# Attention beside an MLP: copies ahead of fades, the second fade of the quads two slots later, y of chunk 0 one slot later

## The reference

```python
# attention: B, H, S, D = 4, 8, 768, 48
f = 1.0 / (1.0 + np.exp(-f_logit))
for t in range(S):
    state = f[:, :, t, :, None] * state + np.einsum('bhd,bhe->bhde', k[:, :, t], v[:, :, t])
    y[:, :, t] = np.einsum('bhd,bhde->bhe', q[:, :, t], state)
# first MLP: x is y as 3072 tokens of 384, w_in 384 x 2048, w_out 2048 x 384
h = x @ w_in
x2 = (h * (1.0 / (1.0 + np.exp(-1.702 * h)))) @ w_out
# second MLP: E = 4 experts, w1 384 x 1024, w2 1024 x 384, p the shares of the experts
for e in range(E):
    out += p[:, e:e + 1] * (np.maximum(x2 @ w1[e], 0.0) @ w2[e])
```

## Time and profile before

| | us |
|---|---|
| median of 3 runs | 1386.29 |
| lowest, highest | 1384.8, 1388.15 |
| the profiled execution, its own time | 1386.22 |
| its span, first to last instruction | 1384.5 |
| TensorE busy, share | 1338.0, 97% |
| VectorE, ScalarE, GpSimd busy | 889.9, 570.7, 635.4 |

### The profile page before, as it was taken

The page is one execution under the profiler, slowest core; times in us unless marked ns, Lnnn a source line. Parts: engine busy times, 40 slices in busy tenths (PEclk is TensorE's granted clock), DMA queues, the critical chain, the costliest instruction groups (busy, mean ns, idle before and its releaser), DMA issues.

```text
span 1384.5 us, 26477 instructions
## 1 busy us (share of the span) xinstructions
PE 1338.0 (97%) x10837; PEld 1239.0 (89%) x10837; DVE 889.9 (64%) x1354; ACT 570.7 (41%) x975; POOL 635.4 (46%) x721
## 2 busy tenths in 40 slices
PE   6889999999999999999999999999999999999999
PEld 5789898989989898998999999999999999999998
DVE  8785848474757565456666666666666666666666
ACT  5564545454544444344333333333323434333331
POOL 8686666665656556466222122121211644444330
PEclk9999999999999999999999999999999999999999
DMA  9535252524343340122101010100101112222111
GB/s 158 120 80 91 69 73 70 71 72 61 82 50 93 41 103 4 63 69 63 35 23 35 13 35 12 35 23 24 35 13 58 46 47 69 70 69 69 57 47 46
DMA packets 240200, 79.34 MB, mean 57 GB/s; under 512 B 189136, under 2 KB 238544, under 8 KB 240080
## 3 DMA queue, kind: packets, MB, share of 16 engines
q1 hardware_dynamic: 201680, 74.11, 22.7%
q10 hardware_dynamic: 38400, 3.55, 2.1%
HBM read 67.83 MB, written 9.78 MB: 56 GB/s over the span
## 4 chain that ended last, share of the span: by engine, by line
PE 79%; DVE 9%; POOL 5%; issue 3%; ACT 2%; DMA 1%; SPq 0%; ACTq 0%; DVEq 0%; POOLq 0%
PE bank L1914 10%; PE bank L1912 10%; PE bank L1913 10%; PE bank L1848 9%; PE bank L1849 9%; PE bank L1847 9%; PE bank L1820 3%; PE bank L1821 3%; PE bank L1822 3%; PE bank L1632 3%; PE bank L1579 2%; PE bank L1577 2%; PE bank L1578 2%; PE bank L1588 2%; POOL g_l L832 2%
## 5 line engine op out<-in xcount | busy, mean ns | idle before, releaser
L1526 DVE SCALAR_TENSOR_TENSOR acc<-bank,p_n,acc 128x384 f32<-128x384 f32 x384 | 234.7, 611 | 68.1 <-PE bank L1914 63.0
L1914 PE MATMUL bank<-w_h,h_l 128*128 128x384 f32 x768 | 257.2, 335 | 0.0
L1912 PE MATMUL bank<-w_h,h_h 128*128 128x384 f32 x768 | 257.0, 335 | 0.0
L1913 PE MATMUL bank<-w_l,h_h 128*128 128x384 f32 x768 | 256.9, 334 | 0.0
L832 POOL TENSOR_TENSOR g_l<-sig,g_h 128x384 fp32r<-128x384 f32 x128 | 151.0, 1180 | 177.6 <-ACT g_h L1084 177.5
L1510 DVE TENSOR_TENSOR bank<-bank,x_copy 128x512 f32<-128x512 f32 x192 | 124.6, 694 | 166.0 <-ACT x_copy L1183 102.6
L1849 PE MATMUL bank<-xs,we_l 128*128 128x512 f32 x528 | 206.4, 391 | 0.0
L1848 PE MATMUL bank<-xs,we_h 128*128 128x512 f32 x528 | 206.2, 391 | 0.0
L1847 PE MATMUL bank<-xs,we_h 128*128 128x512 f32 x528 | 205.5, 389 | 0.6 <-issue 0.6
L882 POOL TENSOR_TENSOR we_l<-we_raw,we_h 128x384 fp32r<-128x384 f32 x96 | 97.1, 1038 | 214.9 <-ACT we_h L1151 214.9
L1183 ACT ACTIVATE x_copy<-bank 128x512 f32<-128x512 f32 x144 | 86.3, 599 | 221.8 <-PE bank L1849 221.5
(11 more groups left out here) (156 smaller groups left out, 2412.3 us busy)
## 6 DMA issues: line engine op xcount, KB each, us to landing
we_raw<-in_moe_w SPq DMA_DIRECT2D x32, 384.0 KB, 4.0
w_raw<-in_moe_w SPq DMA_DIRECT2D x32, 384.0 KB, 3.3
v_sb<-in_v SPq DMA_DIRECT2D x48, 96.0 KB, 2.7
x_dram<-work SPq DMA_DIRECT2D x8, 576.0 KB, 4.9
x_raw<-x_dram SPq DMA_DIRECT2D x12, 384.0 KB, 4.2
f_raw<-in_f_logit SPq DMA_DIRECT2D x56, 72.0 KB, 2.1
q_raw<-in_q SPq DMA_DIRECT2D x56, 72.0 KB, 2.1
k_raw<-in_k SPq DMA_DIRECT2D x56, 72.0 KB, 2.0
```

The source lines that it names most:

```text
L1526: dve.scalar_tensor_tensor(acc[:, pr * TT + i, :], y_bank[y % 3][:, 0:DM], p_n[:, col:col + 1], acc[:, pr * TT + i, :], ALU.mult, ALU.add) ...
L1912: pe.matmul(dst, hh, wh, start=f == 0, stop=False)
L1913: pe.matmul(dst, hh, wl, start=False, stop=False)
L1914: last = pe.matmul(dst, hl, wh, start=False, stop=f == 1)
```

## The change

Nothing is computed differently; instructions move between slots and within them.

1. *Copies of levels.* The copy to `q_split` becomes a step of its own, ("split", L). For levels 3, 4 and 5 it stands at the end of slots 4, 5 and 7, behind sigmoid and `g_h`; before, it stood at the start of slots 5, 7 and 8. Levels 2 and 6 keep their place.
2. *Quads.* The diagonal products become three steps: two ahead of level 2's fade of `k_T` in slot 4, one at the start of slot 5. The sums of odd move from slot 6 to slot 7, behind the mask copies of level 4. The second fade of the quads moves from slot 6 to slot 8. The cross products move from slots 8, 9, 9 to 9, 9, 10, their sums from 8, 9, 9 to 9, 9, 10.
3. *`g_l` last* in slots 4, 5 and 7 as well.
4. *The `k` transpose* of VectorE stands directly behind the `q` transpose, ahead of product 0.
5. *The tail.* Band copies from slot 10 to 11. y and update of the chunks from slots 12, 14, 16 to 13, 15, 16. `k_rows` of chunk 1 from 13 to 14; for chunk 2 it stays in slot 15 on TensorE, behind y 1, and its copy goes to slot 16. The gates' sigmoid from slot 13 and their transpose from slot 14 to the start of slot 15; the decays from 14 and 15 to 15 and 16.

```diff
-    plan[6] = [("quad", "odd"), ("q_fade", 4), ("quad_sum", "odd"), ("quad_fade", 1)]
-    plan[7] = [("level", 4), ("q_fade", 5)]
...
+    plan[7] = [("level", 4), ("split", 5), ("quad_sum", "odd"), ("q_fade", 5)]
+    plan[8] = [("quad_fade", 1), ("level", 5)]
...
-    LOW_LAST = (8, 9)
+    SPLIT_LAST = [("split", L) for L in (3, 4, 5)]
+
+    LOW_LAST = (4, 5, 7, 8, 9)
...
-                if s == "level" and (c >= FIRST or fine(n)):
+                if s == ("level" if fine(n) else "split"):
                     L = c
...
-                        if s != ("level", FIRST) and s[0] != "next_k":
+                        if s[0] != "next_k" and s not in SPLIT_LAST:
                             step(*s, n1, a, b)
-                    if slot == 3:
-                        step("level", FIRST, n1, a, b)
...
-                        if s == "next_k":
+                        if s == "next_k" or (s, c) in SPLIT_LAST:
                             step(s, c, n1, a, b)
...
-                step("transpose", "q", n1, a, b)
+                for t in ("q", "k"):
+                    step("transpose", t, n1, a, b)
                 for slot in range(SLOTS):
                     if slot < FT:
                         gelu_product(n, slot)
-                    if slot == 0:
-                        step("transpose", "k", n1, a, b)
```

More of the change, by code:

```diff
@@ L363, in moe_of_attention_kernel @@
     plan[2] = [("level", 1)]
-    plan[3] = [("quad", "gate"), ("state", 0), ("q_fade", 2)]
-    plan[4] = [("level", 2), ("quad", "diagonal"), ("q_fade", 3)]
-    plan[5] = [("level", 3), ("quad_fade", 0), ("quad_sum", "diagonal")]
-    plan[6] = [("quad", "odd"), ("q_fade", 4), ("quad_sum", "odd"), ("quad_fade", 1)]
-    plan[7] = [("level", 4), ("q_fade", 5)]
-    plan[8] = [("cross", 0), ("level", 5), ("cross_sum", 0)]
-    plan[9] = [("q_fade", 6), ("cross", 1), ("cross", 2), ("level", 6), ("cross_sum", 1), ("cross_sum", 2)]
@@ L371, in moe_of_attention_kernel @@
[L371 to L375, removed]
+    plan[3] = [("quad", "gate"), ("state", 0), ("split", 2), ("q_fade", 2)]
+    plan[4] = [("diagonal_of", 0), ("diagonal_of", 1), ("level", 2), ("split", 3), ("q_fade", 3)]
+    plan[5] = [("diagonal_of", 2), ("level", 3), ("split", 4), ("quad_fade", 0), ("quad_sum", "diagonal")]
@@ new lines, in moe_of_attention_kernel @@
+    plan[6] = [("quad", "odd"), ("q_fade", 4)]
+    plan[7] = [("level", 4), ("split", 5), ("quad_sum", "odd"), ("q_fade", 5)]
+    plan[8] = [("quad_fade", 1), ("level", 5)]
+    plan[9] = [("cross", 0), ("cross", 1), ("split", 6), ("q_fade", 6), ("level", 6), ("cross_sum", 0), ("cross_sum", 1)]
+    plan[10] = [("cross", 2), ("k_rows", 0), ("k_copy", 0), ("cross_sum", 2)]
+    plan[11] = [("state_fade", 0)] + [("band", c) for c in range(CH)]
+    plan[13] = [("y", 0), ("update", 0)]
+    plan[14] = [("state_fade", 1), ("k_rows", 1), ("k_copy", 1), ("x", 0)]
@@ L377, in moe_of_attention_kernel @@
+    plan[15] = [("y", 1), ("update", 1), ("k_rows", 2)]
+    plan[16] = [("state_fade", 2), ("k_copy", 2), ("x", 1), ("y", 2), ("update", 2)]
+    plan[17] = [("x", 2)]
     for r in range(PAIRS):
         plan[11 + r] += [("next_k", r)]
[L379 to L382, removed]
+    plan[15] = [("next_sigmoid", 0), ("next_turn", 0)] + plan[15] + [("next_decays", 0)]
+    plan[16] += [("next_decays", 1)]
@@ L770, in step @@
                     return
-                if s == "quad" and c == "diagonal":
+                if s == "diagonal_of" and not fine(n):
                     pool.wait_ge(qk_quads_loaded, n * 16 * 2 * H)
[L774 to L777, removed]
+                    pool.tensor_tensor(prod[c].rearrange("p (j k d) -> p j k d", j=2, k=QUAD),
+                                       q_quad[:, c, :, :, :], k_quad[:, c, :, :, :], ALU.mult)\
+                        .then_inc(quad_product, 1)
                 if s == "quad" and c == "odd":
@@ L1052, in step @@
                         square(c, i, n)
-                if s == "k_rows" and leads_on(c, a):
+                if s == ("k_rows" if fine(n) else "k_copy") and leads_on(c, a):
                     u = chunk_unit["k_rows", c]
```

## The result

The changed kernel takes **1390.49 us** (median of 8, 1387.08 to 1394.26), the kernel before 1385.78 on the same chips (median of 8, 1383.83 to 1388.15). The ratio is 1.0035, 95% interval 1.002 to 1.0051: slower by 0.35%. Forecast were 1383.5 and a range up to 1390.

A forecast was written before the change was run, and what follows sets the result against it. TensorE, busy 1338.0 of 1384.5 us, was taken as the bound, so only its waits could be won. Waits gone 27.7, new 25.1, net -2.6: from 1386.2 or 1386.3 to 1383.6, stated as 1383.5; range 1373 to 1390.

The forecast's parts named there:

- Level 5's wait: TensorE's wait at level 5 (L1588) for VectorE's mask copies of level 4: 15.3 us over seven intervals, claimed to go.
- level 3's: TensorE's wait of 0.40 us at level 3 in the interval read, claimed to go.
- the step chain to the band: From hidden product 10's start through `g_l` 9 and cross products: last cross sum at +5.85 us, chunk 0's band at +13.66.
- y's wait: New TensorE wait at y of chunk 0, slot 13, for the band copies: 2.2 us an interval, 15.4 over seven.
- Level 6: A wait there for a copy to `q_split` was named as a sign of error; reached 0.4 us after its copy, no term.
- `g_l` 3 and 4, and the first interval: Waits left at slots 4 and 5: 7 x 0.45 = 3.2 us, and 1 more in the first interval.
- Clock falls: Falls of the clock: three before, three after, the new wait being as long as the old; term 0.
- restarts: A restart after a TensorE wait costs 0.1 us more: 3 us gone, 2 us new.
- k loads: ScalarE's four loads from slot 11, now beside the band's stores: 0.3 us in each of six intervals, 1.8 together.
- the long bands: In two of seven intervals the way from last cross sum to band copies was 1.1 us longer: 1.7 counted.
- Rival 2: Slower: the band's wait worse at its stores and load, k loads at 1.1 us, more clock falls: 1393 us; chance 0.2.
- the forecast's swap of one wait for the other: The wait at level 5 goes, one at y of chunk 0 comes: 1380 to 1387 us; chance 0.65.

The follow-up runs named there:

- experiment 1: Changed kernel with the third pair of cross products ahead of `g_l` 9 on GpSimd in slot 10: 1370.32 us, ratio 0.9883 to the kernel before.
- experiment 4: Kernel before the change with only the `k` transpose moved ahead of product 0: 1380.88 us, ratio 0.9957.
- experiment 2: Changed kernel with ScalarE's loads of k's blocks one slot later (slots 12 to 15): 1390.0 us, ratio 1.003 to the kernel before.
- experiment 3: Changed kernel with ScalarE's loads of k's blocks two slots later (slots 13 to 16): 1389.13 us, ratio 1.001 to the kernel before.
- experiment 6: Experiment 1's kernel with VectorE's last cross sum also ahead of product 10: 1366.03 us, ratio 0.9853 to the kernel before.
- experiment 7: Experiment 1's kernel with the `q_split` copies of levels 3 to 5 back at slot starts: 1371.0 us, ratio 0.9884 to the kernel before.
- experiment 8: Experiment 1's kernel with slots 4 and 5 (diagonal products, `g_l` order) as before the change: 1367.02 us, ratio 0.9864 to the kernel before.
- experiment 9: Changed kernel with the edits of experiment 6 and experiment 8 joined: 1362.59 us, ratio 0.9832 to the kernel before.
- experiment 10: Experiment 9's kernel with the `q_split` copy for level 6 ahead of level 5's squares: 1364.34 us, ratio 0.9845 to the kernel before.
- experiment 5: Changed kernel with quads from slot 6 on and tail as before; level copies, diagonal parts and `k` transpose stay: 1372.9 us, ratio 0.9905 to the kernel before.

## Why the prediction was wrong

**What held.** TensorE's waits bound the intervals, and experiments 1 and 4 moved the time by moving them. Level 5's wait went, as did level 3's in intervals 1 to 6. The cross products' new place and the step chain to the band (5.83 for 5.85) are as worked out, and no wait came at y 2. The total of y's wait (18.8 for 18.9) is right too, but partly by luck, as shown below.

**The steps that failed** lie in the sum, not in the mechanism. The profiled execution stands at 1387.1 where the sum had 1383.6, 3.5 more:

- *Level 6, counted at nothing: 3.4.* This is the step that failed. The prediction named a wait there as what would be wrong, "level 6 is reached 0.4 after its copy", and gave it no term. Before, the margin was 0.33 to 0.35 in the four intervals whose clock didn't fall (1.0 to 1.4 in the others), but it stood on the very wait that was taken away. Level 5 and what follows, interval 2, before and then after:

```profile
240.31 0.52 ACT L1084 ACTIVATE g_h<-sig 128x384 fp32r<-128x384 f32 x1 [0.94 <-DVE sig L1421]
240.95 1.84 PE L1588 MATMUL bank<-q_split,k_T 128*32 128x64 f32 x48 [2.12 <-DVE scores_T L1384]
241.64 2.33 ACT L974 ACTIVATE scores_T<-bank 32x256 f32<-32x256 f32 x6 [0.81 <-PE bank L1588]
244.00 1.71 ACT L1049 ACTIVATE q_split<-q_T 48x768 f32<-48x768 f32 x2
```

```profile
240.25 1.53 PE L1586 MATMUL bank<-q_split,k_T 128*32 128x64 f32 x48
240.36 0.49 ACT L1078 ACTIVATE sig<-bank 128x384 f32<-128x384 f32 x1 [1.48 <-PE bank L1577]
240.87 0.52 ACT L1085 ACTIVATE g_h<-sig 128x384 fp32r<-128x384 f32 x1
241.30 2.31 ACT L975 ACTIVATE scores_T<-bank 32x256 f32<-32x256 f32 x6
243.64 1.72 ACT L1050 ACTIVATE q_split<-q_T 48x768 f32<-48x768 f32 x2
```

  Before, ScalarE did sigmoid 8 and `g_h` 7 while TensorE waited for level 5, and began level 5's squares 0.69 after its start. Now level 5 starts at once, both stand ahead of the squares, and these begin 1.05 after; the copy is done 5.11 after level 5's start instead of 4.76. TensorE comes to level 6 after 4.88 instead of 5.11. So 0.35 of margin less 0.35 less 0.23 leaves the copy 0.23 late, and TensorE starts 0.25 behind its end: 0.48. The experiments agree: level 6 waits wherever level 5's wait is gone (1 to 3 and 6 to 10), and nowhere in 4 and 5, where level 5 waits 2.1 and 1.3.
- *`g_l` 3 and 4, and the first interval: 5.2 for 4.2.* The first interval has 0.99 at level 3 and at output 4 each, 0.56 at output 3 and 0.38 at output 15, the others 0.20 and 0.56 at output 3 in turn.
- *Clock falls: four for three, 1.4.* The term of 0 rested on the wait being as long as the old one; it is longer (2.55 to 2.96 in the first six intervals, for 2.1).
- *Against them, restarts: 2.6 better than counted.* An interval less its waits is some 0.5 shorter than before. Level 5 alone, from its start to output 6, is 1.47 in an interval at full clock where it had been 1.78 behind its wait. And 0.3 of the 3.5 lies ahead of the first interval, which starts at 62.98 instead of 62.68.
- *y's wait* came out right only in total. Without k loads it is 14.5 (experiment 3) for 15.4; the k loads cost 4.3 for 1.8, since 0.3 was too little (0.5 to 0.9 an interval); and the long bands cost nothing for 1.7: no interval after was longer by their 1.1 on top (6.87 to 7.27). Rival 2 had the place, with 1.1 for the price. The Trainium skill (DMA: Bandwidth & Descriptors, Issuing engines are not separate DMA queues), which it cited, has the DMAs of all engines interleave on the same 16 DMA engines. The way of 7.1 against 6.4 agrees with it.

**The median lies 3.4 above the profiled execution.** The mean granted clock of the eight runs is 0.991, that of the kernel before on the same chips 0.994. One fall, 3.4 us at half clock, is 0.0012 of it, so these runs have on average some two falls more than before, 3 us: the second half of rival 2. The profiled execution has one more, so by this estimate falls make 1 to 1.6 of the 3.4. Single runs don't follow the clock closely (1390.33 and 1390.64 at 0.993, 1387.08 at 0.992), and no trace of a slower one exists; what else differs in them stays open. So the result, slower by 0.35%, is the forecast's swap of one wait for the other, with level 6 and the clock on top of it. The chance of 0.15 for slower was too small: half of rival 2's price was more clock falls, and the sum counted these at zero although three were already in the trace.

**What was not seen.** Each part was weighed as given, and the sum rightly found the swap nearly even. The experiments show how uneven the parts are: `k` transpose alone -5.3; with copies, diagonals and `g_l` order -13.3; then quads and tail +18; and with the third cross product ahead of `g_l` 9 all of it is -15.8 against before.

## What to carry to other kernels

A margin that was read behind a wait may go with the wait: another engine had used the time too. Here level 6 had 0.35 to spare while TensorE stood 2.1 us ahead of level 5, and waited 0.48 when it no longer did. Such a margin must also be read at full clock; behind a fall it was 1.0 to 1.4. When a step is moved later, look at what stands ahead of it in its new slot on its own engine; here one instruction behind a `g_l` it doesn't need cost 20 us. And when two gains share a cause, as the `k` transpose and the diagonals did, try the smaller edit alone.

## What the runs showed of the hardware

- Loads of 0.4 us each in ScalarE's queue lengthen a chain of small stores and a small load in SyncE's by 0.5 to 0.9 of 6.3 us, beside the stores or beside the load.
- TensorE's granted clock fell to half right behind some waits and not behind others of the same length (0.56 behind 2.79, 1.00 behind 2.96). Of the like waits of 2.0 to 3.0 us at one place of the seven intervals (level 5 before and in experiment 4, y of chunk 0 after and in experiments 2 and 3), three to five were followed by a fall in each profiled execution.
- In the six kernels whose waits at y of chunk 0 were short (experiments 1 and 6 to 10) no wait up to 1.7 inside an interval was; one of 1.72 in experiment 5 was. Longer single waits in the first interval went either way: 2.29 (experiment 7) was, 2.34 and 2.48 (experiments 7 and 10) weren't. The executions of these six have mean clocks of 0.994 to 0.998.
- A fall cost 1.35 to 1.4 us, so a wait of 2 us can cost more than half its length again.
